# One core of a Trainium2 chip: the channel tile of r and k loaded as 128 rows where 112 were loaded

## The reference

```python
B, H, S, D = 4, 8, 768, 48                       # batch, heads, tokens, head size
for t in range(S):                               # layer 1: a linear recurrence per (b, h)
    cur = einsum('bhd,bhe->bhde', u[None] * kt, vt)
    y[:, :, t] = einsum('bhd,bhde->bhe', rt, state + cur)
    state = w[None, :, :, None] * state + einsum('bhd,bhe->bhde', kt, vt)
x = y.transpose(0, 2, 1, 3).reshape(B * S, H * D)         # 3072 tokens x 384
# layer 2: soft mixture of 8 experts with 4 slots each
logits = x @ phi
d = softmax(logits over the tokens); c = softmax(logits over the slots)
slot_out = relu((d.T @ x) @ w1[e]) @ w2[e]       # per expert; w1 384x1024, w2 1024x384
x = c @ slot_out
# layer 3: feed-forward of width 2048
h = x @ w_in; g = h * sigmoid(1.702 * h); out = g @ w_out
```

## Time and profile before

| | us |
|---|---|
| median of 3 runs | 424.57 |
| lowest, highest of them | 420.70, 428.93 |
| the profiled execution | 421.9 |
| its span, first to last instruction | 420.1 |
| mean granted TensorE clock in it | 0.972 of full |

### The profile page before, as it was taken

The page is one execution under the profiler, slowest core; times in us unless marked ns, Lnnn a source line. Parts: engine busy times, 40 slices in busy tenths (PEclk is TensorE's granted clock), DMA queues, the critical chain, the costliest instruction groups (busy, mean ns, idle before and its releaser), DMA issues.

```text
span 420.1 us, 9085 instructions
## 1 busy us (share of the span) xinstructions
PE 393.8 (94%) x3234; PEld 312.6 (74%) x3234; DVE 234.0 (56%) x399; ACT 188.2 (45%) x432; POOL 125.7 (30%) x113
## 2 busy tenths in 40 slices
PE   5759989898988699999999999999999999999996
PEld 4648877777867584457788888888888888888885
DVE  7545667766555623014865565565555655655651
ACT  1124434342434141337666645555464464455552
POOL 5767888876665513002533000000000000000000
PEclk9588999999999879999999999999999999999999
DMA  7899999999999993998000200010020001002002
GB/s 231 243 281 309 295 289 290 285 277 272 272 276 272 365 373 103 353 407 289 2 1 0 76 1 0 3 74 0 0 75 0 0 36 39 0 0 75 2 0 75
DMA packets 28245, 62.39 MB, mean 149 GB/s; under 512 B 2640, under 2 KB 16576, under 8 KB 27840
## 3 DMA queue, kind: packets, MB, share of 16 engines
q1 hardware_dynamic: 27232, 61.61, 48.0%
q10 hardware_dynamic: 992, 0.49, 0.6%
HBM read 57.37 MB, written 4.72 MB: 148 GB/s over the span
## 4 chain that ended last, share of the span: by engine, by line
PE 62%; DVE 2%; ACT 1%; issue 1%; DVEq 0%
PE bank L564 15%; PE bank L565 15%; PE bank L566 15%; PE bank L551 5%; PE bank L490 3%; PE bank L471 3%; PE bank L311 1%; DVE glo L793 1%; PE bank L355 1%; PE bank L532 1%; DVE gf L787 0%; PE bank L376 0%; PE bank L481 0%; PE bank L349 0%; PE bank L435 0%
## 5 line engine op out<-in xcount | busy, mean ns | idle before, releaser
L787 DVE TENSOR_TENSOR gf<-bank,sg 128x512 f32<-128x512 f32 x96 | 66.3, 692 | 86.2 <-ACT sg L938 85.8
L564 PE MATMUL bank<-glo,whi 128*128 128x512 f32 x288 | 112.5, 391 | 0.2 <-DVE glo L793 0.2
L566 PE MATMUL bank<-ghi,wlo 128*128 128x512 f32 x288 | 112.2, 390 | 0.0
L565 PE MATMUL bank<-ghi,whi 128*128 128x512 f32 x288 | 112.2, 389 | 0.0
L938 ACT ACTIVATE sg<-bank 128x512 f32<-128x512 f32 x96 | 57.3, 598 | 94.0 <-PE bank L551 93.9
L793 DVE TENSOR_TENSOR glo<-gf,ghi 128x512 fp32r<-128x512 f32 x96 | 69.4, 723 | 0.2
L564 PEld LDWEIGHTS bank<-glo,whi 128*128 128x128 f32 x288 | 54.1, 188 | 12.2 <-DVE glo L793 1.1
L566 PEld LDWEIGHTS bank<-ghi,wlo 128*128 128x128 f32 x288 | 54.1, 188 | 11.3
L565 PEld LDWEIGHTS bank<-ghi,whi 128*128 128x128 f32 x288 | 54.1, 188 | 11.1
L944 ACT ACTIVATE ghi<-gf 128x512 fp32r<-128x512 f32 x96 | 60.0, 625 | 0.9 <-DVE gf L787 0.9
L830 ACT ACTIVATE yt<-bank 112x512 f32<-112x512 f32 x24 | 14.3, 597 | 83.5 <-PE bank L355 83.5
(11 more groups left out here) (121 smaller groups left out, 403.4 us busy)
## 6 DMA issues: line engine op xcount, KB each, us to landing
ring<-w SPq DMA_DIRECT2D x24, 512.0 KB, 9.0
rkb<-rk SPq DMA_DIRECT2D x24, 448.0 KB, 8.7
krb<-kr SPq DMA_DIRECT2D x24, 384.0 KB, 7.3
ring<-w SPq DMA_DIRECT2D x4, 1536.0 KB, 15.3
ring<-w SPq DMA_DIRECT2D x8, 768.0 KB, 8.8
vb<-v SPq DMA_DIRECT2D x24, 192.0 KB, 7.6
out<-ob SPq DMA_DIRECT2D x18, 256.0 KB, 2.1
ring<-win SPq DMA_DIRECT2D x3, 1024.0 KB, 14.2
```

The lines of the kernel that those rows point to most:

```text
L564: pe.matmul(o, w_hi, lo, start=(f == 0), stop=False)
L565: pe.matmul(o, w_hi, hi, start=False, stop=False)
L566: pe.matmul(o, w_lo, hi, start=False, stop=(f == KF - 1)).then_inc(prod_ps, 1)
L787: dve.tensor_tensor(gf[:, f % 2, :], bank[f % 4][:, :], sg[:, f % 2, :], ALU.mult).then_inc(gf_ok, 1)
```

## The change

SP loads the rk tile of a step as 128 rows of the array, beginning at the step's first row, 112n, into all 128 partitions of `rkb`. The last 16 of them are the first 16 rows of the next step's data. They land in partitions 112 to 127, and nothing reads them. The last step, n = 23, has no rows behind it in the array and is loaded as before. Arithmetic, waits, buffers and the order of the loads are the same, and the host stores the same array.

```diff
+        rk_rows = rk.rearrange("c b p x h t -> (c b p) x h t")
...
                 wait(sp, rks_ok, n - 1)
-                sp.dma_start(rkb[0:PAIR, b % 2, :, :, :], rk_v[n]).then_inc(rk_in[b % 2], 16)
+                if isinstance(n, int) and n == B * C - 1:
+                    sp.dma_start(rkb[0:PAIR, b % 2, :, :, :], rk_v[n]).then_inc(rk_in[b % 2], 16)
+                else:
+
+                    sp.dma_start(rkb[:, b % 2, :, :, :], rk_rows[bass.ds(n * PAIR, P)]).then_inc(rk_in[b % 2], 16)
```

## The result

| | before | after |
|---|---|---|
| median of the runs made together, us | 426.75 (4 runs, 420.7 to 432.2) | 407.94 (4 runs, 407.5 to 409.0) |
| the profiled execution, us | 421.9 | 407.5 |
| its span, us | 420.1 | 405.7 |

What follows compares the result with a forecast made beforehand. The prediction took the full DMA queue, slowed by 112-row rk loads, as the bound, with TensorE close behind. 7.0 + 2.5 + 1.2 + 0.9 = 11.6 us off 421.9 gave 410.3, scaled to 413; range 405 to 422.

Steps and rivals of the forecast that it cites:

- the kr loop: In the recurrence: kk frees krb's half, the next kr loads, GpSimd works back to kk; 10.6 us for two steps.
- The rate: DMA queue in the recurrence: 370 GB/s once rk loads have 128 rows, with bounds of 277 and 385.
- no gain: rk loads: the slow rate belongs to rk's data or the memory mix; 6.0 us slower, about 430.6 us; chance 0.10.
- The share: DMA queue between 40 and 120 us: its share falls from 1.03 to about 0.85.
- waits in the loop: From 40 to 140 us: 7.0 of TensorE's 7.9 us of idle time goes.
- waits in the first steps: TensorE's waits for rks (1.52 us) and the mask (1.77 us): 2.5 of 3.3 us goes.
- waits in the last steps: TensorE's wait of 2.76 us at 146.05 us: 1.2 us of it goes.
- clock: Clock falls at 28 and 144 us, after TensorE sat idle: 0.9 us comes back.
- The rival's price: Scale before the scores, 0.14 us of slack: half the steps lose that, 2.5 us; about 419 us; chance 0.26.
- the clock helps more: Both clock falls vanish and all waits go: 17.5 us gained, about 407 us against the median; chance 0.14.

Runs made afterwards that it cites:

- half-w1 runs: w1 loads of half the columns, in the kernel before and in the changed kernel: 411.6 us and 408.5 us.
- the loads alone: A kernel that only loads, 12 loads to a stage, with the load's shape varied: 112 rows of rk moved 241 GB/s, 128 rows 390.
- the cut of w1: The changed kernel with each w1 load cut into 112 and 16 rows: 427.1 us; as a control into 64 and 64: 445.8 us.
- the stages of rk with kr: In a kernel that only loads, 12 loads of rk and 12 of kr in turn: 42.7 us with 112 rows, 29.2 with 128.
- the second kernel of loads: Loads only, with the destination partitions varied: 112 rows moved 250 GB/s, 128 rows 364, 64 neighbouring rows 210, 64 on every second partition 307.

## Why the prediction was right

**What bounds the kernel.** Right. The queue was full and slow because of rk's shape, and the kr loop passed it on. The half-w1 runs show the first, the loads alone and the cut of w1 the second, the waits the third.

**The rate.** I took 370 GB/s for a queue of 128-row loads, from the earlier trace rows. The loads alone moved 364 to 390 for rk and for rk with kr. The choice between 277 and 385 was right, and so was leaving the rival of "no gain" at a small chance: its premise, 8/7 of the time for 8/7 of the rows, is the opposite of what happened (1.34 us for 1.90).

**The share.** Wrong in size: 0.85 forecast, 0.93 to 0.97 seen. 320 GB/s at a share of 0.93 are 344 at a full one, not 370, and a step takes 0.93 x 5.09 = 4.7 us of the queue, not 4.4. Why the mix in the kernel moves less than the stages of rk with kr was not tried. kr's landing, forecast at 4 to 6 us, is 5.3.

**The terms of the sum**, by the stretches above:

| term | forecast | measured |
|---|---|---|
| waits in the loop | 7.0 (of 7.9) | 7.4 (7.92 to 0.52), step 5 to 23 |
| waits in the first steps | 2.5 (of 3.3) | 0.7 (11.69 to 10.99) |
| waits in the last steps | 1.2 | 1.1 (3.21 to 2.13) |
| clock | 0.9 | 4.6 (2.2 in the first steps, 2.4 in the last) |
| busy time in the loop, same clock | 0 | 0.7 |
| sum | 11.6 | 14.4 by the spans (14.5 by these rounded rows) |

The loop's term was held back for a limit that did not come: scale on VectorE (L638 before, L643 after) had 0.14 us of slack in the earlier trace rows, and I left room for it. From 40 to 120 us TensorE waits 0.36 us in all, and scale itself waits for TensorE. (The rival's price was too high even so: half of 24 steps by 0.14 us are 1.7 us, not 2.5.) The step was misread too: I counted 15 steps in 80 us, 5.3 us each with 5.0 of work. Steps 5 and 23 lie 99.67 us apart, which is 5.54 a step, with 91.75 / 18 = 5.10 of work. The step of 5.09 after is that work.

The mis-sized term is the clock. My 0.9 us was the price of one block of 16 matmuls: L355 took 1.95 us at 31.51, where the granted clock was 0.50, and 1.08 at 65.38, where it was 1.00. That price held: the like of the first took 1.08 us in the changed kernel, at 30.20. But in the first steps two errors nearly cancelled. There I forecast 2.5 us of waits and 0.9 of clock, 3.4 together, and 2.9 came; but 0.7 of it is waits and 2.2 clock, so that the total is near is luck. TensorE's wait for rks fell (at 27.62 us it was 1.52; the same block at 26.39 has none), but the wait for the mask, which I had put down to krb, did not: 1.77 became 2.06, and all such waits of the first 40 us went from 3.6 to 4.8. The clock gave more than the one block that I counted, since the blocks from 28.71 to 34.97 all ran at half clock, wholly or in part (granted 0.50 from 28.8 to 35.6 us). And the second profile of the changed kernel has only 1.1 us here: in it a fall of the clock near 30 us is left (0.83 from 30 to 40 us, for 1.00 in the first profile).

In the last steps the wait was right to 0.1 us: 1.48 is left of 2.76. But I gave the clock no return there. Before, TensorE's granted clock was 0.50 from 144.9 to 151.7 us: the blocks at 146.05 and 149.74 take 1.95 us and their like in the changed kernel 1.08, and two shorter blocks between them lost 0.4 each, 2.6 in all. Both falls were gone in the first profile, which I had put at 0.14 in "the clock helps more". That rival was half right: the clock came back, the waits did not all go.

**The time.** 413 forecast, 407.9 measured, inside the range of 405 to 422. Of the 5 us, 2.8 are the sum's (14.4 for 11.6). The rest is scaling: 407.5 is near the median of the changed kernel, while the 421.9 that I scaled by 1.006 was far under the middle of the kernel before. I had carried the scatter of the kernel before over to the changed one. What makes that scatter is not shown: the cut of w1 at 112, whose queue was full as well, spread by 3.9 us only.

## What to carry to other kernels

When a DMA queue is full, look at the rate in GB/s beside the share: where a full queue moves 280 GB/s and elsewhere in the same trace 370, look for a load of bad shape in it; here the loads beside it paid too. Try filling all 128 partitions with each large load, even with rows that nobody reads: here 14% more bytes took 29% less time. It paid only where the queue was full, since alone both shapes landed after 3.5 us, and it paid by the idle time of the next engine, here 7.4 us in 18 steps. Where TensorE also ran at half clock around its waits (here a granted clock of 0.50 twice, for 6.8 us each), price the clock as its own term: it gave 4.6 us of the 14.4, and most of what scattered from one profile of the changed kernel to the next (busy time 26.99 and 28.25 us in the first steps, idle time 10.99 and 11.50).

## What was not expected of the hardware

- A load of 64 rows takes nearly as long as one of 128 with twice the bytes: 14.9/12 = 1.24 us against 1.34 in a full queue (1.25 against 1.44 in the second kernel of loads). Cutting one 512 KB load a step into two halves by partitions cost 37 us over 24 steps.
- 120 rows are as bad as 112 (237 and 241 GB/s), so nearly full is not good; of the shapes tried only 128 was.
- Sixty-four rows on every second partition moved 307 GB/s, on 64 neighbouring ones 210.
- In the last steps of the changed kernel TensorE kept its full clock (granted 1.00 from 129.59 to 147.00 us) around a wait of 1.48 us; before, the granted clock was 0.50 from 144.9 to 151.7 us, beginning within a wait of 2.76 us. The length of the wait alone does not decide it: the kernel before with half of w1 lost the clock after a wait of 1.63 us (granted 0.50 in the block behind it, 1.95 us), the changed one with half of w1 kept it after 1.62 (1.00, 1.08 us). What decides is not shown.

```profile
136.98 1.95 PE L355 MATMUL bank<-at,vb 128*48 128x128 f32 x16 [1.63 <-DVE at L655]
```

```profile
133.55 1.08 PE L360 MATMUL bank<-at,vb 128*48 128x128 f32 x16 [1.62 <-DVE at L660]
```
